# A three-layer pipeline on one core: the Fourier stage and the norm of the next batch moved into the network of this one

## The reference

```python
for t in range(S):                       # layer 1: gated linear attention, per head
    state = alpha[:, :, t, :, None] * state + k[:, :, t] outer v[:, :, t]
    y[:, :, t] = q[:, :, t] @ state
x = y with the heads side by side        # [4, 768, 384]
mixed = real(fft(fft(x, axis=1), axis=2))            # layer 2
u = x + mixed
un = (u - mean(u)) / sqrt(var(u) + 1e-6)
x = u + relu(un @ w_ch1) @ w_ch2                     # 384 -> 1536 -> 384
h = relu(x.T @ w_tok1) @ w_tok2                      # layer 3: over tokens, 768 -> 256 -> 768
u = x + h.T
out = u + relu(u @ w2_ch1) @ w2_ch2
```

## Time and profile before

| | us |
|---|---|
| median of three runs | 990.28 |
| the profiled execution's own time | 993.23 |
| its span, first to last instruction | 991.4 |
| TensorE matmul rows busy | 941.7 |
| DVE busy | 458.8 |
| ACT busy | 253.1 |
| POOL busy | 172.8 |

### The profile page before, as it was taken

One profiled execution on the slowest core, in us unless ns is written; L12 is line 12 of the kernel. 1 busy time (PEld: TensorE's weight loads), 2 busy tenths in 40 slices (PEclk: granted clock), 3 DMA queues, 4 the chain that ended last, 5 costly groups with the idle time before them and its releaser, 6 DMA issues.

```text
span 991.4 us, 16182 instructions
## 1 busy us (share of the span) xinstructions
PE 941.7 (95%) x5716; PEld 894.5 (90%) x5716; DVE 458.8 (46%) x1099; ACT 253.1 (26%) x641; POOL 172.8 (17%) x282
## 2 busy tenths in 40 slices
PE   4688899999899998899998999999999999999998
PEld 3567899998899998899997999899999999999998
DVE  5466765655855646855556222522142233314222
ACT  2323332224322223322233422321122112211111
POOL 3481222110212111211101331200020010002000
PEclk9999999999899999899998999999999999999999
DMA  8824002323022213023001600200010001000000
GB/s 239 247 49 94 3 5 45 72 49 74 1 49 43 53 27 74 2 49 73 1 11 53 217 24 20 101 1 24 24 48 0 24 24 48 24 0 24 0 24 24
DMA packets 14250, 48.70 MB, mean 49 GB/s; under 512 B 1664, under 2 KB 5888, under 8 KB 12480
## 3 DMA queue, kind: packets, MB, share of 16 engines
q1 hardware_dynamic: 13056, 41.88, 16.0%
q10 hardware_dynamic: 544, 2.36, 1.3%
q0 software_dynamic: 576, 3.55, 1.1%
HBM read 38.35 MB, written 9.44 MB: 48 GB/s over the span
## 4 chain that ended last, share of the span: by engine, by line
PE 85%; DVE 5%; DMA 4%; issue 3%; ACT 1%; POOL 1%; SPq 0%; ACTq 0%; DVEq 0%; POOLq 0%
PE bank L1092 17%; PE bank L1094 15%; PE bank L1093 15%; PE heads L1094 7%; PE heads L1093 7%; PE heads L1092 7%; PE bank L1133 4%; PE heads L1108 4%; PE bank L1137 2%; DMA vt<-v 2%; PE bank L1144 2%; DMA raw_a<-w_ch 1%; PE bank L1099 1%; PE heads L1202 1%; PE heads L1307 1%
## 5 line engine op out<-in xcount | busy, mean ns | idle before, releaser
L937 DVE SCALAR_TENSOR_TENSOR hl<-bank,hh 128x384 fp32r<-128x384 f32 x192 | 106.9, 557 | 333.4 <-ACT hh L572 333.4
L572 ACT ACTIVATE hh<-bank 128x384 fp32r<-128x384 f32 x192 | 94.4, 492 | 306.0 <-PE bank L1094 306.0
L1092 PE MATMUL bank<-nh,w1h 128*128 128x384 f32 x288 | 108.3, 376 | 2.3 <-DVE nl L895 2.1
L1094 PE MATMUL bank<-nh,w1l 128*128 128x384 f32 x288 | 100.0, 347 | 0.0
L1093 PE MATMUL bank<-nl,w1h 128*128 128x384 f32 x288 | 100.0, 347 | 0.0
L1092 PE MATMUL bank<-u2h,w3h 128*128 128x384 f32 x288 | 97.9, 340 | 0.5 <-DVE u2l L1048 0.2
L1094 PE MATMUL bank<-u2h,w3l 128*128 128x384 f32 x288 | 97.4, 338 | 0.0
L1093 PE MATMUL bank<-u2l,w3h 128*128 128x384 f32 x288 | 97.0, 337 | 0.0
L424 POOL TENSOR_TENSOR qkap<-qkap,suf 112x128 f32<-112x128 f32 x96 | 39.8, 414 | 306.1 <-DVE suf L703 299.7
L466 POOL TENSOR_TENSOR u<-u,x2l 128x384 f32<-128x384 f32 x24 | 23.6, 1012 | 288.8 <-DVE u L1069 288.8
L499 ACT ACTIVATE dec<-st,suf 112x96 f32<-112x96 f32 x80 | 30.1, 377 | 166.9 <-DVE st L685 106.8
(11 more groups left out here) (185 smaller groups left out, 2017.2 us busy)
## 6 DMA issues: line engine op xcount, KB each, us to landing
qkap<-qka SPq DMA_DIRECT2D x26, 432.0 KB, 7.0
raw_a<-w_ch SPq DMA_DIRECT2D x6, 768.0 KB, 13.1
mid<-u SPq DMA_DIRECT2D x8, 576.0 KB, 2.9
raw_b<-w_ch SPq DMA_DIRECT2D x6, 768.0 KB, 5.5
xr<-mid SPq DMA_DIRECT2D x8, 576.0 KB, 4.1
out<-u SPq DMA_DIRECT2D x8, 576.0 KB, 2.7
vt<-v SPq DMA_DIRECT2D x14, 288.0 KB, 7.4
qkap<-qka ACTq DMA_DIRECT2D x4, 432.0 KB, 8.1
```

The costliest lines, as they stand in the source:

```text
L572: act.activation(hh[:, s % 4, :], bank[s % 2][:, 0:HALF], ACT.Relu).then_inc(s_hhi, 1)
L937: dve.scalar_tensor_tensor(out=hl[:, s % 4, :], in0=bank[s % 2][:, 0:HALF], scalar=0.0, in1=hh[:, s % 4, :].bitcast(F32), op0=ALU.max, op1 ...
L1092: pe.matmul(out_ap, wh, rh, start=first, stop=False)
L1094: return pe.matmul(out_ap, wl, rh, start=False, stop=last)
```

## The change

- **Order.** Each network is now 48 slots (`SLOTS`), alternately `mlp_in` and `mlp_out`; the last two `mlp_out` of a batch move into slots 1 and 3 of the next. Slots 0 to 30 but six (`PAUSES`) hold one attention step of the next batch each (`VISIT`), at most one per slot where there was one per two. Slots 31 to 47 hold the Fourier stage and norm of the next batch (`tail`); the norm of its last three row tiles comes in slots 3, 7 and 14 of its own network. Only batch 0's Fourier stage stands alone. `u` has two buffers. Loops over batches are written out.
- **Columns folded.** Before F1, DVE adds and subtracts column d and 384 - d (`fold`). Of the six F1 groups two keep 384 columns, the others have 192 or 194; F2 has seven groups of 6 matmuls.
- **Whole-array attention.** ACT copies q into a buffer `qz` with zeros in the other head's rows (two copies a step), and one matmul of 256 columns gives both heads' scores. `dec` is written in two head blocks over zeros (two ACT instructions), and k'v is one matmul of 96 columns.
- **Mirrors by DMA.** SP stores the second half of x to DRAM, copies it there in reversed row order, and loads it into `u`. The flip matmuls and their copies go.
- **Loads.** The pads of q, k and decay come with the data in one DMA of 112 partitions instead of memsets. Four unit buffers serve batch 0, all loaded before the weights, all by SP. Table loads start at steps 3 to 6, weight splits at 6 (ACT) and 8 (POOL).

```diff
+SLOTS = 2 * MLP
+PAUSES = (1, 3, 7, 14, 21, 28)
+VISIT = dict(zip([h for h in range(31) if h not in PAUSES], range(-1, STEPS)))
+SUMS_AT = 31
+F1_AT = 33
+V_AT = {40: 0, 41: 1, 43: 2}
+U_AT = {40: 0, 42: 1, 44: 2}
+MIDDLE_AT = 41
+NORM_AT = {45: (0, 1), 46: (2,)}
+LATE_NORM_AT = {3: 3, 7: 4, 14: 5}
+STD_AT = 42
...
+            def load_mirrors(a):
+                u = us[a % 2]
+                sp.wait_ge(s_x, STEPS * (a + 1))
...
+                sp.dma_start(x_rows[0:HALF].rearrange("(c p) n -> p c n", p=P), x[:, KT:NC, :]).then_inc(s_xrows, 16)
+                sp.dma_start(x_rows[HALF:HALF + 1], x[0:1, KT, :]).then_inc(s_xrows, 16)
+                sp.wait_ge(s_xrows, 32 * (a + 1))
+                sp.dma_start(x_back.rearrange("r (h n) -> h r n", h=2),
+                             x_rows[HALF:0:-1].rearrange("r (h n) -> h r n", h=2)).then_inc(s_xback, 16)
+                sp.wait_ge(s_xback, 16 * (a + 1))
+                sp.dma_start(u[:, 1:NC:2, :], x_back.rearrange("(j p) n -> p j n", p=P)).then_inc(s_mirror, 16)
...
+            def visit(a, k):                              # ACT
+                attn_krt(a, k + 1)
+                attn_qz(a, k + 2, 0)
+                attn_decay(a, k + 1)
+                if k >= 0:
+                    attn_x(a, k)
+                attn_qz(a, k + 2, 1)
...
+            def fold(a):                                  # DVE
...
+                dve.wait_ge(s_x, a * STEPS + STEPS)
                 for part in range(2):
+                    x_sum(part, slice(EARLY, DM)).then_inc(s_xs, 1)
+                for part in range(2):
+                    r = slice(part * KT, (part + 1) * KT)
+                    dve.wait_ge(s_xs, 2 * a + part + 1)
+                    dve.tensor_tensor(xf[:, r, 1:192], tmp[:, r, 1:192], tmp[:, r, 383:192:-1], ALU.add
+                                      ).then_inc(s_fold, 1)
+                    if part == 0:
+                        dve.wait_ge(s_xs, 2 * a + 2)
+                        dve.tensor_copy(xf[:, :, 0:256:255], tmp[:, :, 0:193:192]).then_inc(s_fold, 1)
+                    dve.tensor_tensor(xf[:, r, 192:255], tmp[:, r, 1:64], tmp[:, r, 383:320:-1], ALU.subtract
+                                      ).then_inc(s_fold, 1)
+                    dve.tensor_tensor(xf[:, r, 256:384], tmp[:, r, 64:192], tmp[:, r, 320:192:-1], ALU.subtract
+                                      ).then_inc(s_fold, 1)
...
+                if h == SLOTS - 1 and a + 1 < B:          # DVE, tail: last slot
+                    for i in range(2):
+                        extreme(a + 1, 0, i)
+                    for k in range(2):
+                        prep(a + 1, k)
...
             def attn_scores(a, k):                        # TensorE
-                buf, cols = qkap[k // NC % 2], slice(k % NC * P, (k % NC + 1) * P)
-                pe.wait_ge(s_qk, a * (2 * STEPS) + 2 * k + 2)
-                for h in range(2):
-                    r = slice(64 * h, 64 * h + D)
-                    mm = pe.matmul(score_banks(a, k)[:, h, 0:P], buf[r, 1, cols], buf[r, 0, cols], start=True, stop=True)
-                mm.then_inc(s_sc, 1)
+                buf, cols = chunk(a, k)
+                pe.wait_ge(s_qz, 2 * (a * STEPS + k) + 2)
+                pe.matmul(score_bank(a, k)[:, 0:2 * P], buf[0:PR, 1, cols],
+                          qz[0:PR, k % 2, :, :].rearrange("p h t -> p (h t)"), start=True, stop=True).then_inc(s_sc, 1)
...
+            def visit(a, k):                              # TensorE
+                if k < 0:
+                    pe.wait_ge(s_ua, a * UA)
+                else:
+                    pe.wait_ge(s_at, a * STEPS + k + 1)
+                if k + 1 < STEPS:
+                    attn_turn(a, k + 1)
+                    attn_scores(a, k + 1)
+                if k >= 0:
+                    pe.wait_ge(s_x, a * STEPS + k)
+                    attn_back(a, k)
...
+            for b in range(B):                            # TensorE
+                for h in range(SLOTS):
+                    s = h // 2
+                    if h % 2 == 0:
+                        if s % NF == 0:
+                            pe.wait_ge(s_nlo, b * NC + 3 * (s // NF) + 3)
+                        mlp_in(b, s, w1h, w1l, nh, nl).then_inc(s_hp, 1)
+                    elif s >= 2:
                         mlp_out(b, s - 2, w2h, w2l, s_x2, b * NC + X2_PRIMED)
+                    elif b:
+                        mlp_out(b - 1, MLP - 2 + s, w2h, w2l, s_x2, (b - 1) * NC + X2_PRIMED)
+                    if h in LATE_NORM_AT:
+                        norm(b, LATE_NORM_AT[h])
+                    if b + 1 < B:
+                        if h in VISIT:
+                            visit(b + 1, VISIT[h])
+                        tail(b + 1, h)
```

More of the change, by code:

```diff
@@ L38 @@
 FW = DM // 2 + 2
+GW = HALF + 4
 NU = H // 2
@@ L397, in _ @@
+            sp.wait_ge(s_ua, UA * B)
+            store_mid(B - 2, 1)
+            for i in range(NB_):
+                if i == NB_ - 1:
+                    sp.wait_ge(s_mid, MID_PRIMED + 32 * (B - 1))
+                load_weight(NA + i)
+            store_mid(B - 1, 0)
             load_x2(0)
@@ L610, in _ @@
-            fourier_norm(B - 1, False)
-            for t in (4, 5):
-                norm_rows(B - 1, t)
-            for s in range(MLP):
-                if s % 3 == 2 and s // 3 < NW4:
-                    for half in range(2):
-                        weight_hi(2 * (NA + s // 3) + half)
-                hidden(B - 1, s)
-                if s == 1:
-                    for t in range(3, NC):
-                        norm_split(B - 1, t)
+            for h in range(SUMS_AT, SLOTS):
+                tail(0, h)
@@ new lines, in _ @@
+            for b in range(B):
+                for h in range(SLOTS):
+                    s = h // 2
+                    if h == 4 and b:
+                        mlp_sum(b - 1, 1)
+                    if h == 28:
+                        mlp_sum(b, 0)
+                    if h == 0:
+                        for t in range(3, NC):
+                            norm_stats(b, t)
+                        norm_var(b, 1)
+                    if h % 2 == 0:
+                        hidden(b, s)
+                    if h == 1:
+                        for i in range(6):
+                            norm_scale(b, 1, i)
+                        norm_rows(b, 3)
+                    if h in LATE_NORM_AT:
+                        norm_split(b, LATE_NORM_AT[h])
+                    if b + 1 < B:
+                        if h in VISIT:
+                            visit(b + 1, VISIT[h])
+                        tail(b + 1, h)
@@ new lines, in sums, with f2_v @@
+            def sums(out_ap, terms):
+                for n, (slot, m, table) in enumerate(terms):
+                    mm = three(out_ap, gh[:, slot, m], gl[:, slot, m], csh[:, table, :], csl[:, table, :], n == 0, n == 1)
+                return mm
+            def f2_v(a, j):
+                if j == 0:
+                    pe.wait_ge(s_glo, (a + 1) * (2 * KT))
+                elif j == 1:
+                    pe.wait_ge(s_vc, a * 3 + 1)
+                else:
+                    pe.wait_ge(s_ua, a * UA + 4)
+                m = slice(j * P, (j + 1) * P)
+                sums(bank[(5, 5, 7)[j]][:, 0:FW], ((2, m, 2), (3, m, 3))).then_inc(s_v, 1)
@@ L1281, in _ @@
+            for s in range(MLP - 2, MLP):
+                mlp_out(B - 1, s, w2h, w2l, s_x2, (B - 1) * NC + X2_PRIMED)
             pe.wait_ge(s_wlo, 2 * (NA + NW4 + 1))
```

904 lines of the change are left out of this document (422 added, 482 removed).

## The result

The changed kernel takes 1006.96 us (median of 4 runs, 1005.34 to 1007.63) against 990.75 us (990.18 to 994.17) for the kernel before in the same session: ratio 1.0154, 95% interval 1.0127 to 1.0180. It is 1.5% slower; 983 was forecast, with a range of 960 to 1003. The profiled execution took 1007.35 us, its span 1005.5 (984.8 forecast).

A forecast was written before the change was run, and what follows sets the result against it. TensorE's matmuls, busy 941.7 of 991.4 us, were taken as the bound. 92.5 + 17 + 30.2 + 398 + 77 = 614.7, with the last network's 370.1 a span of 984.8, gave 983 us; range 960 to 1003.

The forecast's parts named there:

- The start: Batch 0's attention: scores wait for both qz halves, full step 4.3 us, net +17 us, bounds 0 and +25.
- The chain: From k'v through state, dec, x and qz to scores: 1.35 us, exposed in the start, hidden in network visits, margin 0.18.
- the first rival: Start not chained, ACT's order costs nothing: minus 16, 967 us; chance 0.17, shared with no interleaved stalls.
- The matmuls: Sign: 84 F2 matmuls and 24 flip records fewer, and half of the 704 scores and k'v records.
- The last network: Last batch's network: full, not touched by the change, 370.1 us.
- DVE's order: Interleaved batches: TensorE stalls 2.1 us at a batch's end (4.4 for the first) and 1.3 at each fold.
- The mirrors: First Fourier stage: three stores and loads take about 11.4 us and hide, being needed 17.4 us after x.
- The rival: Slow mirror turn: few engines move the reversed copy, first stage waits 7 to 13 us; 990, up to 1005; chance 0.22.
- The last batch: Last batch's network: 432 matmuls at 0.175 plus norms 1.2, 77 us.
- every visit misses its slot: Interleaved visits: chain over 1.53 us stalls some 57 visits by 0.32, 18 us, total 1001; chance 0.19.
- Whole-array matmuls: Scores and k'v across both heads, per attention step: bounds -0.10 to +0.16 us, taken as 0.
- my 20: Three interleaved batches: TensorE stalls from DVE's order, 6.1 + 2 x 3.5 + 3.9 + 3 = 20 us.

The follow-up runs named there:

- the order altered there alone: Changed kernel with ACT writing both qz halves before dec and x in batch 0's attention only: 975.4 us, ratio 0.9849.
- the run with eight pieces: Changed kernel with its reversed DRAM mirror copy cut in 8 pieces per row instead of 2: 1000.0 us, ratio 1.0094.
- qz first: Changed kernel with ACT copying both halves of qz before scaling the state and copying x, in all batches: 955.57 us, ratio 0.9645.
- the fastest version: Changed kernel with eight-piece copy, both qz halves first, weight loads before the mid store, earlier x split in DVE's fold and earlier DVE reductions: 936.79 us, ratio 0.9463.
- the run with one more instruction: Changed kernel with an extra one-column ACT copy between dec and x in every attention step: 1012.32 us.

## Why the prediction was wrong, step by step

**What held.** *The start*: +17 forecast, +17.8 measured, by the mechanism named. The size came out by luck. The full step was 4.61 us, not 4.3, since the chain was longer (some 4 us more in all); the first `attn_back` came at 11.4, not 13.6, and the two errors largely cancel. The chain itself costs twice what the first rival put on it (16 us): with the order altered there alone, the start takes 77.9 us instead of 110.35, which is also 15 less than before, a gain that the sum didn't have. *The matmuls*: their records fell from 5716 to 5256, by 460, which is the 84, 24 and 352 that were forecast. *The last network* was as counted. *DVE's order* at the fold and at a batch's start costs TensorE what the chain of waits said, if less: with both put right the three interleaved batches go from 380.1 us to 372.5.

**The mirrors, mis-sized (+7.1).** The step read "The mirrors ... 576 KB took 2.9 us, so three with issue take about 11.4 and hide." That row (`mid<-u`) is a store from SBUF, no measure for a reversed copy within DRAM with an outermost dimension of two: 15.2 us on two engines. The rival had named this place and priced it at 7 to 13 us; the run with eight pieces gives 7.0, and the stage its forecast length. The forecast should have taken the rival's value: no row stood against it.

**The last batch, missed (+12.9).** The step read "The last batch: 432 x 0.175 + norms 1.2 = 77." 7.6 us of the miss are SP's order, shown by the run: a store moved behind sums that now come in slot 4, with the weight loads behind it. I followed PE, DVE and ACT through the new slots, and SP's queue for the mirrors alone. 3.2 us more are 18 matmuls of batch 2's last two `mlp_out`, which the diff moves into this batch and which I had left in the batch before (18 x 0.175, worked out; not tested). Some 2 us are waits not followed up.

**The chain, mis-sized, and its place misjudged.** The step read "this chain of 1.35 us ... has a slot of 1.58 plus a transpose 0.11 to hide in: margin 0.18 us." Measured: second dec 0.36 us after the first instead of 0.24, x 0.36 after it instead of 0.24 to 0.28, qz 0.28 after x instead of 0.13, and 0.08 from state to dec instead of 0.03; with the rest as counted 1.8 us. That is above the 1.69 us from which the rival "every visit misses its slot" decides, and that rival described what happens: 0.29 us in a visit, 18 us forecast for it, 19.1 measured. (1.84 less the 1.53 that fit in a slot and its transpose is 0.31. That the two totals lie so close is in part chance: 57 visits were counted at 0.32, and in the second network 14 pitches lost 0.32 to 0.77 each.) For the handovers on ACT I had taken 0.13 to 0.28, with one pair of rows behind them (dec to x, 0.28), though the margin was an eighth of the sum.

**Whole-array matmuls, on the good side and out of bounds.** "Bounds for a step: -0.10 to +0.16; I take 0." Inside the network k'v now starts 0.27 us after the state matmul and the next matmul 0.14 after k'v (the visit with qz first, above), 0.35 and 0.23 before: -0.17 us a step, and the run with k'v by head again gives back 0.16. TensorE's busy time in the fastest version is 121.6 to 122.9 us a batch, where I had 126: 10.6 us less in three batches, and k'v by head again takes 9.7 of them back. With qz first and DVE's order as forecast the batches take 380.1 us, 12.7 over those 367.4, so the stalls were some 7 us smaller than my 20; which of them, no run tells. The two together paid for the 19 us of the chain. The 398 us for the three batches were right by that accident.

**In sum.** 7.3 + 12.9 + 1.2 + 0.8 - 1.6 = 20.6 of the 20.7 us. Two of three rivals had come true together with the forecast's mechanism, though I had given them 0.22 and 0.19 as if each excluded the rest; 990 and 1001 each stood below the upper end of 1003, their sum with the forecast (983 + 7 + 18 = 1008) above it. That 1008 is so near to the 1007 measured is chance again: it holds neither the 12.9 us of the last batch nor the 17 to 18 that the interleaved batches gave back. (The proportion in the forecast's last step turns a span of 984.8 us into 983.7, not 983, which changes nothing.) With the three causes mended the change is worth 5%, and with DVE's order 5.4%.

## What to carry to other kernels

An engine whose list is in order turns a copy that could be ready early into part of a chain: put what the next step's matmul needs ahead of what waits for this step's result, here worth 51 us of 1007. When sums or stores are moved to a later place, follow every queue that waits for them to the work that stands behind, the one that issues loads too. Where a step's margin is smaller than the spread of the rows that make up its sum, count it as missed; and rivals that don't exclude each other add up in the range.

## What the hardware showed that I had not expected

- **ACT's pitch.** Before, x started 0.28 us after a dec of 0.38, as if the two overlapped by 0.1. Here dec (0.33) to dec and dec to x take 0.36, x (0.25) to the second head's qz 0.28. In the run with one more instruction, x starts 0.11 after a copy of 0.20. The number of partitions doesn't decide it: a weight cast behind x, both on all 128 partitions, starts 0.13 us after an x of 0.23 in the kernel before (26.07 and 26.20), and 0.28 after an x of 0.25 in the run with qz first (30.00 and 30.28). The Trainium skill (ScalarE: Activation LUTs, What ACT_TABLE_LOAD costs) states that back-to-back instructions overlap by about 93 ns; the pairs of the kernel before and the one behind the added copy agree, those of the chain in the changed kernel don't. Why is open; no run here tried it.
- **Pieces and engines.** A DRAM copy of 576 KB took 10.0 us as 384 pieces of 192 bytes for each of eight engines, and 10.3 as 384 pieces of 96 bytes for each of sixteen. As 384 pieces of 768 bytes for each of two it took 15.2. Between 96 and 192 bytes the number of pieces for one engine counted, and not their size.
- **Shapes of the array.** A k'v of two heads on 48 columns each costs 0.16 us more than one of 96 columns across them inside the network, and 0.15 in the usual full step of batch 0's attention without a cast on ACT, where matmuls last nearly twice as long.
